# Eight experts ordered by token count, each place with its own matmul width, and weight loads issued ahead of the stores

## The chip, the cores and the metric

One core of a Trainium2 chip runs the whole program. The metric is device time in microseconds (us) of that core; the kernel is timed in several runs, and one more execution is recorded by the hardware profiler. TensorE is called PE here, its weight loads PEld, VectorE DVE, ScalarE ACT, GpSimd POOL, and SyncE, which only issues DMAs, SP.

## What is computed

Three stages follow each other. (1) Retention: for 4 batches, 8 heads, 576 positions and head size 64, decayed scores times `v`; the result is read as N = 2304 tokens of D = 512. (2) A mixture of 8 experts with one expert per token:

```python
e_idx = np.argmax(x @ w_gate, axis=1)
for e in range(E):
    mask = e_idx == e
    h = np.maximum(x[mask] @ w1[e], 0.0)      # 512 -> 1024
    out[mask] = gate_w[mask, None] * eom[mask, e, None] * (h @ w2[e])   # 1024 -> 512
```

(3) A bilinear layer: `((x @ w_a) * (x @ w_b)) @ w_out`, 512 to 1536 to 512.

With the reference's inputs the router's argmax gives the experts 0 to 7 these numbers of tokens: 259, 313, 335, 290, 273, 287, 292, 255 (2304 in all).

## The kernel before

**Precision.** Every f32 product is made of three products of rounded operands: a tile is split in a high part (`w_hi`, `x_hi`, `h_hi`, written by ACT) and the rest (`w_lo`, `x_lo`, `h_lo`, written by DVE), and PE does hi by hi, hi by lo and lo by hi into one PSUM bank.

**Routing (before the experts).** While the retention runs, every token gets a rank within its expert. A table of slots then holds, expert after expert, the token numbers in blocks of R = 112. The experts' columns are worked off in *windows*: a window is up to W = 3 x 112 = 336 tokens of one expert. DVE counts how many windows each expert needs (`count` against `full`, `n_win`, L1354 to L1356), sums them to `starts` (the first window of each expert, L1361 to L1364), and works out for each window its first slot (`win_slots`) and its first output column (`win_cols`, L1377 to L1391). PE, ACT, DVE, POOL and SP read `starts` into registers, and loop over the windows of each expert; a window's number of columns is always 336, whether or not the expert fills it, and what is computed too much is overwritten by the next window's result. With the counts above every expert needs one window, so there are 8; they are numbered from 0.

**The experts.** The loops go over pairs of experts (`pair_of_experts`, L465), since the weights have two buffers, s = 0 and 1. For window b of expert e:

- PE (`body`, L1885): first layer, 8 blocks f of the hidden size, 4 blocks d of D, three products each: 96 matmuls of 336 columns (L1895, L1903 for the first three f, which are interleaved, and L1913 for the other five), then the second layer, 96 more (L1924). Behind blocks 2 to 5 of the second layer it transposes the next window's tokens, three transposes each (`turn_window`, L1869), into `px`. Before transposing block d it waits for `x_lo` of block d - 1. Block f of the first layer uses the bank of block f - 3, and waits for `h_lo` of that block.
- ACT (`body`, L945) and DVE (`body`, L1427) each run one fixed order: five blocks of `h_hi` (L954) / `h_lo` (L1436); then, in turn, one unit of the *next* expert's weights (`w_hi`, L950 / `w_lo`, L1431, 1024 columns) and one of the remaining three blocks, and a fourth unit; then four more units in turn with the next window's `x_hi` (L931) and `x_lo` (L1406). DVE's unit in that part comes behind its `x_lo`, ACT's comes ahead of its `x_hi`. Last come one part of the bilinear weights, which each window prepares on the side (L977, L1414 to L1425), and the copies of the result to `y_out` (L981, L1461), after which `y_kept` lets SP store and PE write `py` again.
- SP (`body`, L651): when window b has begun, it asks for the 8 units of the next expert's weights (512 KB each, L604), waits until the prepared bilinear weights of the last window are stored, and loads the next raw ones (L622); then it stores the window's token numbers (L669), waits for `y_kept` at the window's end, stores `y_out` (L674) and, once DVE has finished them, the prepared bilinear weights (two DMAs of 896 KB, L628).
- POOL gathers the tokens of the window after the next one from DRAM (L802) when the transposes have freed `x_blk`.

The last expert's window (`last_experts`, `last_body`) has a body of its own, in which ACT and DVE prepare the input of the bilinear stage instead of weights. The first expert's weights are loaded and split during the retention (`first_units`, `first_low`, L1284).

**The bilinear stage** is fully written out: 18 steps, products of 384 columns (L1979) and an output part of 512 columns (L2004).

Of the kernel before, what the change touches and what calls it, by code (L numbers as in the profile page):

```python
# [5 lines left out]
def retention_table(heads, seq, chunk, scale):  # L6
# [10 lines left out]
    return np.stack([q, k], 1)[..., order].reshape(chunk, 2, chunks * heads).astype(np.float32)  # L17


def retention_moe_bilinear(nc, q, k, v, w_gate, w_output_gate, w1, w2, w_a, w_b, w_out, out):  # L20
# [5 lines left out]
    i32 = mybir.dt.int32  # L26
    u32 = mybir.dt.uint32
    ALU = mybir.AluOpType
# [18 lines left out]

    R = 112
    WB = 3
    W = WB * R  # L50
    NJ = -(-N // W)
    NW = (N + E * (W - 1)) // W
    NB = WB * NJ
# [35 lines left out]
    CONSTS = 27  # L89
# [8 lines left out]
    gate_dram = nc.dram_tensor("gate_of_token", (N, 1), f32, kind="Internal").ap()  # L98
    powers_dram = nc.inline_tensor(retention_table(H, S, P, DH ** -0.5), name="decay_powers").ap()
# [3 lines left out]
    with ctx:  # L103
# [55 lines left out]
        starts = sb("starts", [1, E + 2], i32)  # L159
        win_cols = sb("win_cols", [1, NW1], i32)  # L160
# [18 lines left out]
        n_win = sb("n_win", [P, E], on=phase)  # L179
# [12 lines left out]
        full = sb("full", [P, NJ], on=phase)  # L192
# [25 lines left out]
        count = sb("count", [P, E, NJ], on=phase)  # L218
        st_f = sb("st_f", [P, E + 1], on=phase)
        st_x = sb("st_x", [P, E + 1, E], on=phase)  # L220
# [98 lines left out]
        powers_in = sem("powers_in")  # L319
        const_in = sem("const_in")  # L320
# [135 lines left out]
        def expert_windows(eng, e, s, b0, body):  # L456

            body(e, s, b0, True)
            b1 = eng.value_load(starts[0:1, bass.ds(e + 1, 1)], min_val=1, max_val=NW - 1 + s)
            with eng.If(b1 > b0 + 1):  # L460
                with eng.Fori(b0 + 1, b1) as b:
                    body(e, s, b, False)
            return b1

        def pair_of_experts(eng, e, body):  # L465

            b = eng.value_load(starts[0:1, bass.ds(e, 1)], min_val=0, max_val=NW - 1)
            for s in range(2):
                b = expert_windows(eng, e + s, s, b, body)

        def experts(eng, body):

            with eng.Fori(0, E // 2) as pair:
                pair_of_experts(eng, pair * 2, body)


        def last_experts(eng, body, last_body):

            b = eng.value_load(starts[0:1, E - 2:E - 1], min_val=0, max_val=NW - 1)
            b = expert_windows(eng, E - 2, 0, b, body)  # L480
# [53 lines left out]
        def _(sp):  # L534
# [116 lines left out]
            def body(e, s, b, first):  # L651

                if first:
# [3 lines left out]
                    for u in range(UE):  # L657
                        load_unit(e + 1, 1 - s, u)
# [1391 lines left out]
```

## Time and profile before

| | |
|---|---|
| median of 3 runs | 791.69 us (790.98 to 793.42) |
| the profiled execution's own time | 791.41 us |
| its span in the trace | 789.6 us |
| PE busy | 776.4 us, 98% of the span |
| PEld / DVE / ACT / POOL busy | 718.6 / 479.3 / 282.0 / 78.8 us |
| experts, first matmul to last | 121.1 us to 368.6 us of the span |

The page gives for each engine its busy time, in 40 slices how busy it was and which clock PE was granted, then the chain of work that ended last, and the costliest groups of instructions. The trace behind it can be asked for single instructions in order of time, for what each waited for, and for sums over a stretch. A PE instruction's listed duration overlaps with the next one's; what counts for the time is the distance from start to start.

### The profile page before, as it was taken

The page shows a single profiled execution, that of the slowest core. Times are in us where ns is not written, and L with a number is a line of the kernel's source. Part 1 is how long each engine was busy: PE and PEld are TensorE (multiplying, and loading weights), DVE is VectorE, ACT ScalarE, POOL GpSimd, SP SyncE. Part 2 cuts the span into 40 slices and gives each one's busy share as a digit, 9 for nine tenths or more (in the row PEclk, how much of TensorE's full clock was granted, in tenths as well). Part 3 has the DMA queues.
Part 4 walks back from the last instruction along what each step waited for, and adds up shares of the span by engine and source line. Part 5 has one row for each costly group of instructions (what it writes and reads, how often), then busy time and mean ns, then how long its engine had stood idle before and what let it go on. Part 6 is the DMA issues. An engine that isn't in the chain of part 4 may idle for free.

```text
span 789.6 us, 15184 instructions
## 1 busy us (share of the span) xinstructions
PE 776.4 (98%) x5483; PEld 718.6 (91%) x5486; DVE 479.3 (61%) x898; ACT 282.0 (36%) x501; POOL 78.8 (10%) x112
## 2 busy tenths in 40 slices
PE   8999999999999999999999999999999999999996
PEld 6888859999999999999899999999999999999994
DVE  5577886655856757656666777654663565444471
ACT  4555644453644544634232233222122222221121
POOL 2000031102102002010002000111100011110002
PEclk9999999999999999999999999999999999999998
DMA  8999738296695695867962458875445556454502
GB/s 180 239 236 244 200 110 262 85 344 216 212 361 176 244 327 176 298 216 260 370 245 81 152 198 345 310 286 202 177 159 210 201 215 238 160 196 149 201 1 80
DMA packets 116594, 169.09 MB, mean 214 GB/s; under 512 B 63965, under 2 KB 83455, under 8 KB 116543
## 3 DMA queue, kind: packets, MB, share of 16 engines
q1 hardware_dynamic: 112223, 157.45, 58.5%
q0 software_dynamic: 4176, 10.92, 4.3%
q8 instruction: 31, 0.51, 0.3%
q14 instruction: 20, 0.16, 0.1%
q10 hardware_dynamic: 144, 0.04, 0.0%
HBM read 131.34 MB, written 37.06 MB: 213 GB/s over the span
## 4 chain that ended last, share of the span: by engine, by line
PE 94%; DMA 2%; POOL 1%; DVE 1%; issue 1%; SPq 0%; ACT 0%; POOLq 0%; DVEq 0%
PE pz L1979 32%; PE po L2004 19%; PE py L1924 15%; PE pu L1913 10%; PE pu L1895 4%; PE pscore L1669 3%; PE pout L1723 2%; PE pu L1903 2%; DMA w_lo<-bilinear_weights 1%; PE pq L1657 1%; PE pq L1683 1%; PE pstate L1711 1%; PE px L1869 1%; PE pk L1657 1%; PE pout L1699 1%; PE pscore L1753 1%
## 5 line engine op out<-in xcount | busy, mean ns | idle before, releaser
L1979 PE MATMUL pz<-x_hi,w_hi 128*128 128x384 f32 x504 | 170.2, 338 | 0.8 <-DMA w_lo<-bilinear_weights 0.8
L1979 PE MATMUL pz<-x_hi,w_lo 128*128 128x384 f32 x504 | 169.6, 337 | 0.0
L1979 PE MATMUL pz<-x_lo,w_hi 128*128 128x384 f32 x504 | 169.2, 336 | 0.0
L1528 DVE TENSOR_TENSOR u<-pz,p 128x384 f32<-128x384 f32 x72 | 40.2, 558 | 115.4 <-PE pz L1979 114.9
L1979 PEld LDWEIGHTS pz<-x_hi,w_hi 128*128 128x128 f32 x504 | 94.5, 187 | 4.3 <-DMA w_lo<-bilinear_weights 1.1
L1979 PEld LDWEIGHTS pz<-x_lo,w_hi 128*128 128x128 f32 x504 | 94.7, 188 | 0.6
L1979 PEld LDWEIGHTS pz<-x_hi,w_lo 128*128 128x128 f32 x504 | 94.6, 188 | 0.0
L1026 ACT COPY p<-pz 128x384 f32<-128x384 f32 x36 | 17.3, 481 | 212.7 <-PE pz L1979 211.0
L1431 DVE TENSOR_TENSOR w_lo<-land,w_hi 128x1024 fp32r<-128x1024 f32 x56 | 68.2, 1217 | 28.9 <-ACT w_hi L950 28.9
L2004 PE MATMUL po<-wo_hi,g_hi 128*128 128x512 f32 x216 | 84.2, 390 | 0.0
L2004 PE MATMUL po<-wo_hi,g_lo 128*128 128x512 f32 x216 | 84.2, 390 | 0.0
L2004 PE MATMUL po<-wo_lo,g_hi 128*128 128x512 f32 x216 | 84.2, 390 | 0.0
L1924 PE MATMUL py<-h_hi,w_hi 128*128 128x336 f32 x256 | 83.7, 327 | 0.0
L1924 PE MATMUL py<-h_hi,w_lo 128*128 128x336 f32 x256 | 81.0, 317 | 0.0
L1924 PE MATMUL py<-h_lo,w_hi 128*128 128x336 f32 x256 | 80.9, 316 | 0.0
L950 ACT CAST w_hi<-land 128x1024 fp32r<-128x1024 f32 x56 | 58.7, 1050 | 26.5 <-DMA land<-in_moe_w_dram 26.5
L1913 PE MATMUL pu<-x_hi,w_hi 128*128 128x336 f32 x160 | 51.5, 322 | 0.0
L1913 PE MATMUL pu<-x_hi,w_lo 128*128 128x336 f32 x160 | 50.7, 317 | 0.0
L1913 PE MATMUL pu<-x_lo,w_hi 128*128 128x336 f32 x160 | 50.6, 316 | 0.0
L1436 DVE SCALAR_TENSOR_TENSOR h_lo<-pu,h_hi 128x336 fp32r<-128x336 f32 x56 | 28.3, 505 | 34.4 <-ACT h_hi L954 33.0
L1041 ACT CAST g_hi<-g 128x384 fp32r<-128x384 f32 x72 | 33.6, 515 | 43.5 <-DVE g L1551 40.2
L1924 PEld LDWEIGHTS py<-h_lo,w_hi 128*128 128x128 f32 x256 | 48.4, 189 | 0.0
(256 smaller groups left out, 1330.7 us busy)
## 6 DMA issues: line engine op xcount, KB each, us to landing
land<-in_moe_w_dram SPq DMA_DIRECT2D x64, 512.0 KB, 8.0
w_hi<-bilinear_weights SPq DMA_DIRECT2D x31, 896.0 KB, 4.6
w_lo<-bilinear_weights SPq DMA_DIRECT2D x31, 896.0 KB, 6.9
bilinear_weights<-w_hi SPq DMA_DIRECT2D x12, 896.0 KB, 6.1
bilinear_weights<-w_lo SPq DMA_DIRECT2D x12, 896.0 KB, 8.2
wo_land<-in_moe_w_out_dram SPq DMA_DIRECT2D x18, 512.0 KB, 3.6
y_columns<-y_out SPq DMA_DIRECT2D x8, 672.0 KB, 5.4
q_in<-in_q_dram SPq DMA_DIRECT2D x32, 128.0 KB, 2.9
```

Of the source, the lines that this page charges most:

```text
L950: nc.scalar.copy(w_hi[1 - s][:, u, :], land[1 - s][:, u, :]).then_inc(hi_done, 1)
L1026: nc.scalar.copy(p1[:], pz[n % 2][:, 0:T]).then_inc(z_kept_act, 1)
L1041: nc.scalar.copy(hi[:, MADE[i], :], g[:, MADE[i], :]).then_inc(g_hi_ready, 1)
L1431: nc.vector.tensor_tensor(w_lo[1 - s][:, u, :], land[1 - s][:, u, :], w_hi[1 - s][:, u, :], ALU.subtract).then_inc(lo_done, 1)
L1436: nc.vector.scalar_tensor_tensor(out=h_lo[:, f, :], in0=pu[f % NPU][:, 0:W], scalar=0.0, in1=h_hi[:, f, :], op0=ALU.max, op1=ALU.subtract) ...
L1528: nc.vector.tensor_tensor(dst, pz[n % 2][:, 0:T], more, ALU.add).then_inc(z_kept_dve, 1)
L1669: last = nc.tensor.matmul(pscore[half][0:r, j, 0:r], kT[d, c, j, 0:r], qT[d, c, j, 0:r], start=True, stop=True)
L1895: last = nc.tensor.matmul(pu[f][:, 0:W], w[s][:, d, at(f)], x_hi[:, d, :], start=(d == 0 and w is w_hi), stop=False)
L1913: last = nc.tensor.matmul(pu[f % NPU][:, 0:W], w, m[:, d, :], start=(d == 0 and n == 0), stop=(d == DC - 1 and n == 2))
L1924: last = nc.tensor.matmul(py[d][:, 0:W], w, m[:, f, :], start=(f == 0 and n == 0), stop=(f == FF - 1 and n == 2))
L1979: ins = nc.tensor.matmul(pz[n % 2][:, 0:T], w, m, start=(k in FRESH and j == 0 and i == 0), stop=(j == DH2 - 1 and i == 2), skip_group_che ...
L2004: ins = nc.tensor.matmul(po[i][:], m[:, c, rows], w_, start=(q == 0 and f == 0 and n == 0), stop=(q == NQ - 1 and f == 1 and n == 2))
```

## The change

Experts are no longer worked off by their number. Each has a *place*: the one whose weights are loaded during the retention, expert 0, comes first, the other seven follow by ascending token count. Each place has a fixed width:

`WIDTH = [320, 272, 288, 296, 300, 304, 320, W]`, with W = 336.

All matmuls of a window, `h_hi`, `h_lo`, `y_out` and the stores of a window have the width of its place instead of 336. The gather, the transposes, and `x_hi` and `x_lo` keep 336. An expert with more tokens than its place's width gets further windows of the same width, each advancing by 224 tokens. DVE works out the places at run time (`key`, `less`, `place_of`, `at_rank`, `by_rank`), with four small tables that ACT's queue loads at the start. The loops over pairs of experts are written out, one body for each place, on all engines.

In SP's order the first 4 units of the next weights now come ahead of the stores of the window before, and the last 4 behind them.

On DVE, one split of a unit (`first_low`) leaves the last batch of the retention (where the fifth row tile's was) and comes behind `starts`; the one behind `starts` and the one behind `gate_t` come behind the `x_lo` of window 0, and PE asks for one unit fewer before its first window.

```diff
+def expert_plan(experts, blocks, widths, step, tokens):
+    order = np.arange(experts)
+    prefer = np.where(order == 0, -8.0 * experts * tokens, order)
+    more = 1 + -(-(tokens - min(widths)) // step)
+    over = np.array([[-1] + [w + step * j for j in range(more - 1)] for w in widths])
...
-    NJ = -(-N // W)
-    NW = (N + E * (W - 1)) // W
-    NB = WB * NJ
+    WIDTH = [320, 272, 288, 296, 300, 304, 320, W]
+    STEP = WB - 1
+    NW = E + -(-(N - min(WIDTH)) // (STEP * R))
+    NB = -(-N // R)
...
             def body(e, s, b, first):
                 if first:
                     sp.wait_ge(began, b + 1)
                     sp.sem_inc(alone_sp, 1)
-                    for u in range(UE):
-                        load_unit(e + 1, 1 - s, u)
-                    sp.wait_ge(stage_stored, e * 32 + 32)
-                    sp.sem_inc(alone_sp, 1)
-                    load_raw((w_a, w_b)[s], e - s, 0, stage_in)
-                    sp.wait_ge(cols_ready, 1)
-                    sp.wait_ge(slots_stored, 32)
+                    expert = sp.value_load(order[0:1, e + 1:e + 2], min_val=0, max_val=E - 1)
+                    for u in range(DC):
+                        load_unit(expert, 1 - s, u)
+                    if e == 0:
+                        sp.wait_ge(cols_ready, 1)
+                        sp.wait_ge(slots_stored, 32)
+                    else:
+                        store_y(e - 1, b - 1)
+                        sp.wait_ge(stage_lo_done, e * 2)
+                        store_w2(e - 1, 0, stage_stored)
+                    for u in range(DC, UE):
+                        load_unit(expert, 1 - s, u)
+                    sp.wait_ge(stage_stored, e * 32 + 32)
+                    load_raw((w_a, w_b)[s], e - s, 0, stage_in)
+                elif e < E - 1:
+                    store_y(e, b - 1)
+                store_ids(e, b)
+                if e == E - 1:
+                    store_y(e, b)
...
-                    unit = None if last and c == TOGETHER else first_units(b, c - 1 if not (last and c > TOGETHER) else c - 2, first, last)
+                    unit = None if last and c >= TOGETHER else first_units(b, c - 1, first, last)
...
-            first_low(UE - 2, UE - 2)
+            first_low(3, 5)
...
-            first_low(UE - 1, UE - 1)
...
             for d in range(DC):
                 turn_window(0, d, py[d])
+            for u in range(UE - 2, UE):
+                first_low(u, u)
...
-            pe.wait_ge(lo_done, UE - 1)
+            pe.wait_ge(lo_done, UE - 2)
             def body(e, s, b):
+                cols_of = slice(0, WIDTH[e])
...
-                            last = nc.tensor.matmul(py[d][:, 0:W], w, m[:, f, :],
+                            last = nc.tensor.matmul(py[d][:, cols_of], w, m[:, f, cols_of],
                                                     start=(f == 0 and n == 0), stop=(f == FF - 1 and n == 2))
```

How the instructions stand on SP, in a window in the middle (`land0` is the buffer of the next expert's weights, `w2_land0`, `w2_hi0` and `w2_lo0` the bilinear weights prepared on the side). Before:

```order
L604 ISA [waits began]
L604 DMA land0<-in_moe_w1_dram 128x1024
...
L604 DMA land0<-in_moe_w2_dram 128x2x512
...
L622 DMA w2_land0<-in_moe2_w_b_dram 128x2x128 [waits stage_stored]
...
L669 DMA token_of_column<-token_of_slot 16x21
L671 ISA [waits y_stored]
L674 DMA y_columns<-y_out 128x4x336 [waits y_kept_act,y_kept_dve]
...
L628 ISA [waits stage_lo_done]
L628 DMA bilinear_weights<-w2_hi0 128x1792
...
L628 DMA bilinear_weights<-w2_lo0 128x1792
```

And now, in window 1:

```order
L703 TENSOR_LOAD order [waits began]
...
L628 DMA land0<-in_moe_w1_dram 128x1024
...
L692 REGISTER_ALU [waits y_kept_act,y_kept_dve]
L692 DMA y_columns<-y_out 128x4x320
L652 DMA bilinear_weights<-w2_hi0 128x1792 [waits stage_lo_done]
L652 DMA bilinear_weights<-w2_lo0 128x1792
...
L628 DMA land0<-in_moe_w2_dram 128x2x512
...
L646 DMA w2_land0<-in_moe2_w_b_dram 128x2x128 [waits stage_stored]
...
L682 DMA token_of_column<-token_of_slot 16x17
```

The stores, which stood ahead of all 8 loads of a window (as the last rows of the window before), now stand between its first 4 and its last 4, and the raw bilinear weights stay last.

On DVE, between the last rank of the retention stage and `starts` (`tokens_of` is in `plog`). Before:

```order
L1354 TENSOR_TENSOR count<-plog,full 128x56
L1356 TENSOR_REDUCE n_win<-count 128x8 [waits dve_step]
L1358 TENSOR_SCALAR slots<-pout 128x3 [waits slots_done,dve_step]
...
L1361 TENSOR_TENSOR st_x<-earlier,n_win 128x72
L1362 TENSOR_REDUCE st_f<-st_x 128x9 [waits dve_step]
L1363 TENSOR_SCALAR starts<-st_f 1x1 [waits dve_step]
L1364 CAST starts<-st_f 1x9
```

And now:

```order
L1404 TENSOR_TENSOR less<-key 1x64 [waits dve_step]
L1407 TENSOR_SCALAR slots<-pout 128x3 [waits slots_done,dve_step]
...
L1410 TENSOR_REDUCE place_of<-less 1x8
L1411 TENSOR_TENSOR at_rank<-win_no,place_of 1x64 [waits dve_step]
L1413 TENSOR_TENSOR by_rank_x<-at_rank,of_expert 1x192 [waits dve_step]
L1415 TENSOR_REDUCE by_rank<-by_rank_x 1x3x8 [waits dve_step]
L1417 TENSOR_TENSOR count<-by_rank,over 1x88 [waits dve_step]
L1418 CAST order<-by_rank 1x8 [waits dve_step]
L1419 TENSOR_REDUCE n_win<-count 1x8
L1420 TENSOR_TENSOR st_x<-earlier,n_win 1x72 [waits dve_step]
...
L1423 CAST starts<-st_f 1x9
```

Ahead of the `slots` three small steps stand where two stood; between the `slots` and `starts` there are seven more steps.

## Rows read from the trace of the kernel before

**Rows 1.** The page: engines, granted clock in 40 slices, chain that ended last.
```profile
PE 776.4 (98%) x5483; PEld 718.6 (91%) x5486; DVE 479.3 (61%) x898; ACT 282.0 (36%) x501; POOL 78.8 (10%) x112
PEclk9999999999999999999999999999999999999998
PE 94%; DMA 2%; POOL 1%; DVE 1%; issue 1%; SPq 0%; ACT 0%; POOLq 0%; DVEq 0%
```

**Rows 2.** Busy time by stage: stretch, its length, busy by engine, PEclk, DMA share, GB/s.
```profile
121.10:368.60 247.50, 247.46 (x1631) 246.00 (x1632) 153.21 (x222) 119.41 (x192) 29.49 (x32) 1.00 0.71 249
```

**Rows 3.** Chain that ended last, window 2: start, us, engine, line, count.
```profile
183.32 3.68 PE pu L1895 x24
187.00 1.84 PE pu L1903 x12
188.84 9.40 PE pu L1913 x60
198.24 5.55 PE py L1924 x36
203.79 0.29 PE px L1869 x3
204.08 1.85 PE py L1924 x12
...
210.52 3.70 PE py L1924 x24
```

**Rows 4.** The same chain in the bilinear stage.
```profile
506.63 8.20 PE po L2004 x36
491.95 14.69 PE pz L1979 x84
```

**Rows 5.** A row of PE's timeline in the retention stage, and its group by form.
```profile
100.02 0.66 PE L1683 MATMUL pq<-ident,xT 128*128 128x128 f32 x4
...
L1683 PE MATMUL pq<-ident,xT 128*128 128x128 f32 x64 | 10.5, 287 | 0.0
```

**Rows 6.** ACT's timeline in window 2 (start, us; idle before and releaser in brackets).
```profile
187.65 0.45 ACT L954 ACTIVATE h_hi<-pu 128x336 fp32r<-128x336 f32 x1 [2.55 <-PE pu L1903]
197.32 1.05 ACT L950 CAST w_hi<-land 128x1024 fp32r<-128x1024 f32 x1 [4.15 <-DMA land<-in_moe_w_dram]
204.12 0.44 ACT L931 CAST x_hi<-px 128x336 fp32r<-128x336 f32 x1 [0.53 <-PE px L1869]
```

**Rows 7.** DVE's timeline, end of window 2 and start of window 3.
```profile
203.06 1.21 DVE L1431 TENSOR_TENSOR w_lo<-land,w_hi 128x1024 fp32r<-128x1024 f32 x1
204.59 0.51 DVE L1406 TENSOR_TENSOR x_lo<-px,x_hi 128x336 fp32r<-128x336 f32 x1 [0.32 <-ACT x_hi L931]
211.46 1.23 DVE L1431 TENSOR_TENSOR w_lo<-land,w_hi 128x1024 fp32r<-128x1024 f32 x1
216.53 0.91 DVE L1461 COPY y_out<-py 128x336 f32<-128x336 f32 x2
219.07 1.12 DVE L1436 SCALAR_TENSOR_TENSOR h_lo<-pu,h_hi 128x336 fp32r<-128x336 f32 x2 [1.63 <-ACT h_hi L954]
```

**Rows 8.** SP's timeline in window 2.
```profile
186.66 0.43 SPq L674 DMA_DIRECT2D y_columns<-y_out  x1
187.99 1.20 SPq L628 DMA_DIRECT2D bilinear_weights<-w_lo  x1
192.74 4.68 SPq L604 DMA_DIRECT2D land<-in_moe_w_dram  x8
```

**Rows 9.** DMA of window 2: total, then stretches as in rows 2.
```profile
DMA packets 3841, 7.94 MB, mean 256 GB/s; under 512 B 320, under 2 KB 1856, under 8 KB 3840
...
188.00:192.00 4.00, 4.00 (x27) 3.87 (x26) 2.03 (x4) 1.46 (x4) 0.00 (x0) 1.00 1.05 401
208.00:214.00 6.00, 6.00 (x43) 5.99 (x42) 4.92 (x9) 2.56 (x4) 1.43 (x3) 1.00 0.00 0
```

**Rows 10.** Timelines of DVE, PE and the chain, end of the routing to the first window.
```profile
105.11 1.21 DVE L1284 TENSOR_TENSOR w_lo<-land,w_hi 128x1024 fp32r<-128x1024 f32 x1
118.27 0.16 DVE L1390 TENSOR_REDUCE early_n<-early 1x1 f32<-1x15 f32 x1
118.46 0.14 DVE L1391 TENSOR_SCALAR first_group<-early_n 1x1 int32<-1x1 f32 x1
119.85 1.23 DVE L1284 TENSOR_TENSOR w_lo<-land,w_hi 128x1024 fp32r<-128x1024 f32 x1
121.04 1.75 DVE L1406 TENSOR_TENSOR x_lo<-py,x_hi 128x336 fp32r<-128x336 f32 x4
...
116.66 3.51 DMA x_blk<-x_tokens,slots
121.14 3.98 PE pu L1895 x24
```

More of the change, by code:

```diff
@@ L17, in retention_table @@
     return np.stack([q, k], 1)[..., order].reshape(chunk, 2, chunks * heads).astype(np.float32)
+def expert_plan(experts, blocks, widths, step, tokens):
+    import numpy as np
+    order = np.arange(experts)
+    prefer = np.where(order == 0, -8.0 * experts * tokens, order)
+    more = 1 + -(-(tokens - min(widths)) // step)
+    over = np.array([[-1] + [w + step * j for j in range(more - 1)] for w in widths])
+    of_expert = np.stack([0 * order, order, blocks * order])
+    by_rank = np.zeros((3, experts + 1))
+    by_rank[2, experts] = blocks * experts
+    return more, [np.asarray(m, dtype=np.float32).reshape(1, -1) for m in (prefer, over, of_expert, by_rank)]
 def retention_moe_bilinear(nc, q, k, v, w_gate, w_output_gate, w1, w2, w_a, w_b, w_out, out):
@@ L1011, in last_body @@
                     act.wait_ge(y_stored, b * 16 + 16)
-                    nc.scalar.copy(y_out[:, d, :], py[d][:, 0:W]).then_inc(y_kept[0], 1)
-            with act.Fori(0, E // 2 - 1) as pair:
-                pair_of_experts(act, pair * 2, body)
-            n_windows = last_experts(act, body, last_body)
+                    nc.scalar.copy(y_out[:, d, 0:w], py[d][:, 0:w]).then_inc(y_kept[0], 1)
+            n_windows = experts(act, body, last_body)
             act.wait_ge(down_done, n_windows * DC)
@@ L1512, in last_body @@
                     dve.wait_ge(y_stored, b * 16 + 16)
-                    nc.vector.tensor_copy(y_out[:, d, :], py[d][:, 0:W]).then_inc(y_kept[1], 1)
-            with dve.Fori(0, E // 2 - 1) as pair:
-                pair_of_experts(dve, pair * 2, body)
-            n_windows = last_experts(dve, body, last_body)
+                    nc.vector.tensor_copy(y_out[:, d, 0:w], py[d][:, 0:w]).then_inc(y_kept[1], 1)
+            n_windows = experts(dve, body, last_body)
             def keep_sum(step, kind, k, dst, more, of):
@@ L1894, in up_first @@
                             for w in (w_hi, w_lo):
-                                last = nc.tensor.matmul(pu[f][:, 0:W], w[s][:, d, at(f)], x_hi[:, d, :],
+                                last = nc.tensor.matmul(pu[f][:, cols_of], w[s][:, d, at(f)], x_hi[:, d, cols_of],
                                                         start=(d == 0 and w is w_hi), stop=False)
```

161 lines of the change are left out of this document (95 added, 66 removed).

## The prediction

> **What bounds the kernel now.** I read the page first [rows 1]: PE is busy for 98% of the span, its granted clock reads 9 tenths or more in every slice but the last (the 2.4 GHz level), and 94% of the chain that ended last is PE. So only work that leaves PE, or a new wait on PE, moves the time. The table by stage [rows 2] gives the experts 247.5 us, 247.46 of them PE busy, over eight windows: 30.9 us each. The chain through one window [rows 3] has nothing but PE: 3.68 + 1.84 + 9.40 + 5.55 + 3 x 1.85 + 3.70 = 29.72 us for 192 matmuls of 336 columns, or 154.8 ns each from start to start, and four groups of transposes of 0.29 us. No other engine holds PE up there: ACT waits 4.15 us for weights in the middle of the window [rows 6] and PE does not notice.
>
> **What a column costs.** The bilinear stage has two more widths on the same chain [rows 4]: 84 matmuls of 384 columns take 14.69 us, 174.9 ns each; 36 of 512 columns take 8.20 us, 227.8 ns each. From 336 to 384 that is 20.1 ns for 48 columns, 0.419 ns each; from 384 to 512, 52.9 for 128, 0.413. One column in one cycle at 2.4 GHz is 0.417, and about 15 ns a matmul are fixed. The three widths lie on one line, so at 336 the columns set the spacing and not the weight load that each matmul has. I extend the line down to 272 columns: 154.8 - 64 x 0.417 = 128.1 ns. The nearest row that says whether loads can follow is four f32 transposes with a 128x128 load each [rows 5]: (0.66 - 0.29) / 3 = 0.123 us apart. A full load every 123 ns has been seen, and 128 is asked.
>
> **The narrower windows.** With the counts of the reference the places hold 259, 255, 273, 287, 290, 292, 313 and 335 tokens, against widths of 320, 272, 288, 296, 300, 304, 320 and 336: each fits, there are still 8 windows. The widths sum to 2436, before 8 x 336 = 2688. That is 252 columns fewer in each of 192 matmuls: 252 x 192 x 0.417 ns = **20.2 us less** (20.0 with 0.413, 20.3 with 0.419). It is all on PE, which is the path. The shortest window falls from 30.9 to 25.8 us.
>
> The Trainium skill speaks against this size: TensorE: Matmul & The Clock Gate, section Back-to-back issue gap, gives a sustained spacing of about 81 ns at 128 columns and 131 ns at 512, 0.13 ns a column. By that the change would be worth 6.3 us. This trace disagrees at 512 columns (227.8 ns), and the sum goes by the trace.
>
> **What now has to fit in a shorter window.** The cover of every transfer and split shrinks by up to 5.1 us. I take window 1 (272 columns), with T its start on PE.
>
> *DVE and ACT, middle.* DVE's splits of a unit (1.23 us) alternate with `x_lo` (0.51), which stay at 336 columns [rows 7]; overlapped starts make that about 1.65 us a round. PE's round there was 1.85 + 0.29 = 2.14 us and becomes 1.83. Tight but covered. In the first layer DVE's round is 1.55 to 1.65 against PE's 1.54; PE asks for these blocks only five blocks later, so I cost it at nothing. Without that cover it would be 0.1 us a block.
>
> *DVE, end.* The bilinear splits and `y_out` follow the last unit. That last unit starts at 211.46 and `y_out` ends at 217.44 [rows 7]; its start is tied to the last transposes, and those come only 60 matmuls ahead of the window's end. With 272 columns 60 matmuls shrink by 1.6 us in all, of which 36 spacings and one round fall ahead of it: the end of `y_out` moves from 3.3 to about 3.9 us behind the next window's start. The first `h_lo` of that window is wanted 4.97 us behind its start now (219.07 against 214.1), about 4.4 with 288 columns. The 1.63 us that DVE waited there shrink to about 0.5, and it still has to read `starts` and branch, which is hidden now. I take 0.1 us for each short window; bounds 0, and 1 us for the three shortest if the branch shows.
>
> *PE's own start.* PE asks for `h_lo` of block 0 after 36 matmuls, and that needs 28 matmuls, ACT (0.45) and DVE (0.51). The 8 matmuls between shrink from 1.24 to 1.02 us while ACT and DVE shrink less (0.45 to 0.41, 0.51 to about 0.43): under 0.1 us a window. With the item above: **+0.5 us** over the stage, bounds 0 and 3.
>
> *The weights.* Before, SP asked for them at T + 9.4 (192.74 against 183.3), behind three stores [rows 8], and the first was used at T + 14 [rows 6]. DMA moves 7.94 MB a window at 401 GB/s when it runs, and stands idle for the last 6 us [rows 9]. If only the width had changed, DVE's fourth split would still end at T + 21 (203.06 + 1.21 [rows 7]) where the next `x_lo` is wanted near T + 17.8, and PE would stand some 2 to 3 us in the narrowest windows. The new order on SP asks for 4 units (2.10 MB) at about T + 1, so the first lands long before ACT wants it (T + 8.4, five blocks in). What is late next is unit 4, behind the stores: what is left of the gather (0.69 MB at most), 2.10, `y_out` 0.66, bilinear stores 1.84 and the unit itself 0.52 make 5.8 MB, 14.5 us at 401 GB/s, so T + 15.5, and T + 13.8 if the gather is over. ACT must have split it (1.05 us) before the `x_hi` behind the first transposes, which come 132 matmuls in: 20.5 us in before (203.79 against 183.32), 17.0 now. So unit 4 is wanted by T + 16.3 in window 1 and between T + 17.2 and 18.9 in windows 2 to 6; units 5 to 7 follow at 1.3 us each where 1.83 us are available. Cost: nothing, with 0.8 us to spare in window 1. The raw bilinear weights wait for the stores (about T + 13.5) and land near T + 21, wanted at T + 25. Each window's work is 7.9 MB or 20 us of DMA, in 25.8 us at the least.
>
> **Routing.** One split of 1.13 us leaves the rank's path [rows 10]; the ranks then wait for PE's logits, so about 0.45 us of it come back, and the gather of window 0 (3.51 us of DMA on the chain) starts that much earlier. DVE gets seven more small steps before `starts`, about 0.2 us each (118.27 to 118.46), +1.4 us, and one more for `hop`; but the split at 119.85 (1.2 us) moves behind `x_lo`. So `x_lo` of window 0 stays at about 121.0, and is first wanted 24 matmuls in; `starts` is wanted by PE at 115.2 and comes at about 115.1, before fillers that the gather outlasts. Sum: **-0.4 us**, bounds -0.8 and +1. The four small loads on ACT's queue at the start come before a table load, and ACT's first real work is at 6.2 us: nothing. Last window and bilinear stage are as before: 0.
>
> **The sum.** 791.41 (the profiled execution) - 20.2 + 0.5 - 0.4 = 771.3. The median is 0.28 above that execution, so 771.6 us. About 0.3% (2.4 us) is what a measurement of this kernel can tell from no change.
>
> **The rivals.**
> 1. *The last four units, or DVE, come too late.* For it: under 1 us to spare in window 1, DVE rounds within 0.2 us of PE's, a stretch of DMA at full rate 20 us long. Against: windows 2 to 6 have 2 to 3 us to spare. If unit 4 lands at T + 17.5 only windows 1 and 2 lose, 1.2 and 0.3 us; at T + 19.5 the six windows lose 11 us. With the DVE bound of 3 us I put this case at 773.5 to 780.
> 2. *The weight load gets a floor below 336 columns.* PEld is listed busy for 246.0 of 247.5 us [rows 2], and no row has such loads at 128 ns behind f32r matmuls; the 123 ns are transposes. A floor of 141 ns, halfway, would cost (12.9 + 6.2 + 2.9 + 1.2) ns x 192 = 4.5 us: 776. A floor at 154.8 would leave nothing: 792. The skill's rule quoted above is of this kind, with a gain of 6.3 us; the line through three widths is against it.
> 3. *Slower: one expert more than fits.* From one token over its place's width an expert runs a second window of that width, 25.8 to 30.9 us, which is more than the 20 gained: 797 to 802. The narrowest margins are 1 token at the last place (where before had the same limit) and 7 to 17 at places 1 to 6; before never counted against these widths, so the trace does not show them. The counts above are exact sums of the reference's choice, and a near tie moves one token or two.
> 4. *The change does not do what it says:* the split order on SP hides nothing because the stores at its middle wait for `y_kept` (T + 3.9). SP is through with its 4 loads at about T + 3.5, so this wait costs 0.4 us of issue while 2 MB are queued: no time of its own.
>
> **How the numbers follow.** The forecast (770.3 to 773.5) gets 0.74, rival 1 0.17, rival 2 0.05 (0.01 of it with no gain), rival 3 0.03, and something faster than 770.3 0.01. Two in ten may stay out; I take 769.7 to 778.0, which holds the forecast, its bounds and most of rival 1. Faster by over 0.3%: 0.96; within: 0.01; slower: 0.03.
>
> **What would show it.** The experts' stretch takes about 227.5 instead of 247.5 us, PE busy all through. On the chain, 60 first-layer matmuls of a 272-column window take 7.8 us (9.40 at 336): a spacing of 128 ns; more means rival 2. ACT's wait for the first unit (4.15 us) is gone, and a wait for `land` may stand at the fifth unit; PE idle at the transposes (`px`) with `x_lo` as the releaser means rival 1. More than 8 x 32 matmuls of each product in the second layer means rival 3. The first window starts near 120.7 us. The forecast is wrong if windows 1 to 4 are longer than 192 x spacing + 1.3 us.

## The result and the profile after

The changed kernel takes 785.65 us (median of 5 runs, 783.74 to 788.01) against 791.69 for the kernel before (790.62 to 793.42), a ratio of 0.9918 (95% interval 0.9891 to 0.9945; intervals stand in brackets from here on). 6 us were gained where 20 were forecast. The profiled execution took 783.74 us; its span is 781.9 us, 7.7 less than before.

The page of the changed kernel: span, engines, granted clock in 40 slices, chain that ended last.

```profile
span 781.9 us, 14929 instructions
PE 760.1 (97%) x5485; PEld 700.4 (90%) x5485; DVE 479.5 (61%) x906; ACT 280.7 (36%) x500; POOL 75.3 (10%) x110
PEclk9999999999999999999999999999999999999999
PE 79%; DMA 10%; SPq 4%; issue 2%; DVE 2%; ACT 1%; POOLq 0%; POOL 0%; DVEq 0%
```

PE's busy time fell by 16.3 us, but PE no longer fills the chain: it was 94% of it [rows 1] and is 79%, and DMA is on it with 10%. The table by stretch has one row for each of windows 0 to 6 (columns as in [rows 2]):

```profile
122.92:152.64 29.72, 29.72 (x204) 29.48 (x205) 20.19 (x30) 14.44 (x24) 4.90 (x7) 1.00 0.57 183
152.64:180.08 27.44, 25.93 (x207) 25.42 (x205) 18.46 (x28) 15.06 (x24) 3.03 (x4) 1.00 0.81 289
180.08:211.03 30.95, 28.68 (x207) 28.28 (x206) 19.45 (x29) 15.00 (x24) 3.34 (x5) 0.94 0.74 254
211.03:239.91 28.88, 27.76 (x206) 27.36 (x205) 19.41 (x29) 15.10 (x24) 3.21 (x4) 1.00 0.77 272
239.91:268.81 28.90, 28.44 (x207) 27.81 (x205) 19.38 (x29) 15.15 (x24) 3.21 (x4) 1.00 0.80 274
268.81:297.97 29.16, 28.25 (x207) 27.85 (x205) 19.42 (x29) 15.17 (x24) 3.22 (x4) 1.00 0.79 271
297.97:329.08 31.11, 29.79 (x206) 29.36 (x205) 19.68 (x30) 15.27 (x24) 3.30 (x5) 1.00 0.73 254
sum 206.16, PE 198.58 PEld 195.55 DVE 135.99 ACT 105.18 POOL 24.22; mean PE 28.37 PEld 27.94 DVE 19.43 ACT 15.03 POOL 3.46
```

Read the length against PE's busy time. In window 0 they are equal. In each of the six others PE stands for 0.5 to 2.3 us, 7.58 in all; before, the same seven windows took 216.65 us, all of them busy. Window 2 also has a granted clock of 0.94 in the mean. The list of PE's waits in these windows has one line (total, times, longest), and it is the sign of rival 1:

```profile
PE px L1934 <- DVE x_lo L1466: 7.5, 6, 2.3
```

What is behind it shows on the chain through window 2 (T = 180.08), and on ACT's timeline:

```profile
186.59 13.56 DMA land<-in_moe_w_dram
...
201.12 0.44 ACT x_hi L975
201.58 0.52 DVE x_lo L1466
202.10 0.04 issue
202.15 0.82 PE px L1934 x3
```

```profile
193.55 1.05 ACT L996 CAST w_hi<-land 128x1024 fp32r<-128x1024 f32 x1
200.16 1.04 ACT L996 CAST w_hi<-land 128x1024 fp32r<-128x1024 f32 x1 [5.57 <-DMA land<-in_moe_w_dram]
201.12 0.43 ACT L975 CAST x_hi<-px 128x336 fp32r<-128x336 f32 x1
```

ACT has split units 0 to 3 by 194.6 and then waits 5.57 us for unit 4, the first behind the stores. The transposes that its next `x_hi` copies were done at 198.3. ACT cannot take them first, because its program has the unit ahead of them; `x_lo` waits for `x_hi`, and PE's second transposes for `x_lo`.

SP's timeline and the DMA by stretch, in the same window:

```profile
181.22 2.48 SPq L628 DMA_DIRECT2D land<-in_moe_w_dram  x4
184.81 0.42 SPq L692 DMA_DIRECT2D y_columns<-y_out  x1
185.28 0.50 SPq L652 DMA_DIRECT2D bilinear_weights<-w_hi  x1
185.84 0.53 SPq L652 DMA_DIRECT2D bilinear_weights<-w_lo  x1
186.59 4.97 SPq L628 DMA_DIRECT2D land<-in_moe_w_dram  x4
```

```profile
180.08:183.10 3.02, 3.02 (x25) 3.02 (x24) 2.82 (x4) 1.62 (x3) 2.07 (x3) 1.00 0.58 119
183.10:186.70 3.60, 3.60 (x28) 3.43 (x27) 2.28 (x6) 1.24 (x3) 0.00 (x0) 1.00 0.95 344
186.70:190.00 3.30, 3.30 (x27) 3.30 (x27) 1.09 (x3) 1.76 (x3) 0.00 (x0) 1.00 1.02 302
190.00:196.00 6.00, 6.00 (x48) 6.00 (x47) 5.83 (x7) 4.05 (x6) 0.00 (x0) 1.00 1.05 400
196.00:200.00 4.00, 3.88 (x30) 3.64 (x29) 0.00 (x0) 0.00 (x0) 0.00 (x0) 1.00 1.02 392
...
202.20:205.50 3.30, 3.30 (x15) 3.30 (x16) 2.66 (x3) 1.74 (x3) 0.00 (x0) 0.50 0.50 135
```

SP asks at T + 1.1 as forecast. The DMA engines are full only from T + 3 (share 0.58 before that, 119 GB/s), and for the next 7 us they move 344 and 302 GB/s although they are full; only then come the 400 of [rows 9]. The last row is the other thing to see: behind the 2.27 us in which PE stood, the granted clock is 0.50, PE's lower level, for 3.3 us.

The rest of the difference lies outside these windows. The first window starts at 122.92 instead of 121.14 [rows 10], and the part from window 7 to the end takes 452.8 us instead of 451.8.

### The profile page after: what moved, and what is told of

It reads as the page before. It is cut to its first block, busy times and chain, and to the rows that moved or that the text cites. A ratio compares the mean times of both kernels' runs of the same rounds, so it can differ in the third digit from the quotient of the medians.

```text
span 781.9 us, 14929 instructions
## 1 busy us (share of the span) xinstructions
PE 760.1 (97%) x5485; PEld 700.4 (90%) x5485; DVE 479.5 (61%) x906; ACT 280.7 (36%) x500; POOL 75.3 (10%) x110
## 4 chain that ended last, share of the span: by engine, by line
PE 79%; DMA 10%; SPq 4%; issue 2%; DVE 2%; ACT 1%; POOLq 0%; POOL 0%; DVEq 0%
PE pz L2047 33%; PE po L2072 19%; DMA land<-in_moe_w_dram 10%; PE py L1992 9%; PE pscore L1734 3%; PE pu L1981 2%; PE pout L1788 2%; SPq L628 2%; PE pq L1748 1%; PE pq L1722 1%; PE pstate L1776 1%; PE px L1934 1%; PE pout L1764 1%; PE pu L1963 1%; PE pk L1722 1%
## 5 line engine op out<-in xcount | busy, mean ns | idle before, releaser
L1992 PE MATMUL py<-h_hi,w_hi 128*128 128x320 f32 (+6 forms) x256 | 80.8, 316 | 0.0
L1992 PE MATMUL py<-h_lo,w_hi 128*128 128x320 f32 (+6 forms) x256 | 77.9, 304 | 0.0
L1992 PE MATMUL py<-h_hi,w_lo 128*128 128x320 f32 (+6 forms) x256 | 77.9, 304 | 0.0
L996 ACT CAST w_hi<-land 128x1024 fp32r<-128x1024 f32 x56 | 58.5, 1046 | 30.1 <-DMA land<-in_moe_w_dram 30.1
L1981 PE MATMUL pu<-x_hi,w_hi 128*128 128x320 f32 (+6 forms) x160 | 49.2, 308 | 0.0
L1992 PEld LDWEIGHTS py<-h_hi,w_hi 128*128 128x128 f32 x256 | 48.8, 191 | 0.0
L1992 PEld LDWEIGHTS py<-h_hi,w_lo 128*128 128x128 f32 x256 | 48.7, 190 | 0.0
L1981 PE MATMUL pu<-x_lo,w_hi 128*128 128x320 f32 (+6 forms) x160 | 48.4, 303 | 0.0
## 6 DMA issues: line engine op xcount, KB each, us to landing
bilinear_weights<-w_lo SPq DMA_DIRECT2D x12, 896.0 KB, 10.7
```

Source lines behind the costliest of these rows:

```text
L996: nc.scalar.copy(w_hi[1 - s][:, u, :], land[1 - s][:, u, :]).then_inc(hi_done, 1)
L1981: last = nc.tensor.matmul(pu[f % NPU][:, cols_of], w, m[:, d, cols_of], start=(d == 0 and n == 0), stop=(d == DC - 1 and n == 2))
L1992: last = nc.tensor.matmul(py[d][:, cols_of], w, m[:, f, cols_of], start=(f == 0 and n == 0), stop=(f == FF - 1 and n == 2))
```

## The experiments

Theory A: unit 4 lands too late for windows this short, and ACT's fixed order hands that on to PE. Rival B: the rounds of DVE or ACT, or the new order itself, are what a short window can't hold. Rival C: the routing and the fillers ahead of the first window (fillers are matmuls on `idle_in` whose results nobody reads; `wait_busy` issues them so that PE does not stand). Rival D: the falls of the clock. A "way" below is the time from the first `slots` on DVE to the first `pu` on PE, 8.38 us before, 9.36 in the changed kernel. The seven windows are windows 0 to 6.

### w336: the old width, all else new

```diff
-    WIDTH = [320, 272, 288, 296, 300, 304, 320, W]
+    WIDTH = [W] * 8
```

> The changed kernel with every place 336 columns wide again, its order of work and its order on SyncE kept. Theory A (the fifth of the eight weight units lands too late for the shortened windows, ScalarE works in a fixed order and holds x_hi back behind it, and PE stands at the transposes): with 30.9 us windows the unit is wanted at T + 20 to 20.5 and lands before, so every window is 30.9 to 31.1 us and PE has no wait there. What is left against the kernel before is the longer routing: first window 0.5 to 2 us later. 791.5 to 793.5 us. Rival B (the new order itself, or the DMA traffic it makes, costs time whatever the width): windows of 31.5 us and more, 795 us and up. Rival C (the start costs nothing by itself): 791 us or less.

794.66 us, ratio 1.0019 [1.0002, 1.0036]. The median lies 1.2 us above the range expected, the windows are as expected. The seven by the table, with no wait of PE in them:

```profile
125.58:342.19 216.61, 216.61 (x1428) 215.31 (x1429) 139.31 (x198) 107.50 (x168) 24.60 (x31) 1.00 0.71 246
```

216.61 us, before 216.65: the new order costs nothing where the window is long. ACT splits unit 4 at T + 18.7 to 20.2 in windows 1 to 6 here too, so the landing is not late because windows are short. It was no earlier in the kernel before, T + 18.9 to 19.9 in the same windows. Its row of window 2 (T = 183.16):

```profile
202.54 1.05 ACT L950 CAST w_hi<-land 128x1024 fp32r<-128x1024 f32 x1 [0.28 <-DMA land<-in_moe_w_dram]
```

Moving units 0 to 3 ahead of the stores brought them forward, but unit 4 has the same stores and the same four units queued ahead of it in either order. 30.9 us had room for that. B falls as far as the order goes. What the kernel pays, about 2 us in the medians (1.5 by the ratio), lies outside the windows: the part from window 7 to the end takes 452.7 us (before 451.8), and the rest is ahead of the first window. In the profiled execution, the slowest of twelve, that window starts at 125.58. PE stood 2.00 us for `starts` ahead of it, and then:

```profile
120.30:123.60 3.30, 3.30 (x11) 1.70 (x10) 2.99 (x16) 0.00 (x0) 0.00 (x0) 0.51 0.29 74
```

The clock falls over the fillers, and the way takes 11.0 us.

### ahead0: all loads behind the stores, as before

```diff
-                    for u in range(DC):
+                    for u in range(0):
                         load_unit(expert, 1 - s, u)
...
-                    for u in range(DC, UE):
+                    for u in range(0, UE):
                         load_unit(expert, 1 - s, u)
```

> The changed kernel with all eight weight loads behind the stores again, as in the kernel before, and the narrow widths kept. Theory A: the units land in the old rhythm, the fourth is split on VectorE near T + 20 to 21, and the next x_lo is wanted at T + 17.8 in the 272-column window; the last four follow about as late as now or a little earlier, since nothing else of the load moves. Windows 1 to 6 are then about as long as now or longer: excess over their columns 8 to 16 us in sum, 783 to 790 us. If the new order on SyncE does all that it is for, this run is over 4 us slower than the changed kernel; if it does nothing, within 2 us of it.

790.96 us, ratio 0.9981 [0.9964, 0.9998], about 5 us over the changed kernel and 1 us above the range expected. The seven windows take 213.15 us, and PE's waits grow:

```profile
PE px L1937 <- DVE x_lo L1469: 11.8, 6, 2.8
```

Now ACT waits 6.02 us for the first unit (window 1, T + 14.4). The change's order on SP, with its loads in two halves, is worth 7 us of windows; without it the narrow columns would have kept 3.5 of the 21.2 us that they save (`early_b` below).

### swap: ScalarE copies x_hi ahead of the unit

```diff
                 for d in range(DC):
-                    high(DC + d)
                     turn_window(b + 1, d, px)
+                    high(DC + d)
```

> The changed kernel with one thing moved on ScalarE: in the rounds of the last four units each x_hi is copied before the unit's rounding, not behind it. Theory A: x_hi no longer waits for the unit of its own round, so a landing up to one round (1.8 us) later is borne; of the 9.6 us by which windows 1 to 6 exceed their columns, about 6 to 8 go, and the longest of PE's waits for x_lo go with them. 776 to 779 us. Rival B (VectorE's rounds of 1.7 us, or PE itself, set the windows): no change, 783 to 786 us. Rival D (a fall of the granted clock to 1.2 GHz makes part of it): 1 to 2 us stay in the window in which it shows.

781.03 us, ratio 0.9851 [0.9827, 0.9876]: 4 to 5 us less from one line. The seven windows take 202.47 us. The expectation of 776 to 779 was missed, since the wait has only moved on by a round:

```profile
PE px L1934 <- DVE x_lo L1466: 5.9, 5, 3.1
```

`x_hi` of the first round is now copied in time, but DVE too has a fixed order, `x_lo` of round 1 behind the `w_lo` of unit 4. And unit 4 was split at T + 20.0 to 20.9, in window 1 at T + 20.9 instead of 18.4. There the first 3 us of DMA moved 117 GB/s and not 196, and the 6 us from T + 6.4 on 353 and not 406. That is 0.56 MB or 1.4 us at 400 GB/s; the rest is not accounted for. `after2` below has T + 19.3 there with the changed kernel itself, so how much of the later landing is due to the moved line is open. Window 6, 320 columns wide, has no wait left.

### early: units 0 to 3 asked for one window earlier

```diff
+            def load_early(e, b):
+                sp.wait_ge(up_done, b * FF)
+                sp.sem_inc(alone_sp, 1)
+                sp.wait_ge(hi_done, e * UE + (UE + DC))
+                sp.sem_inc(alone_sp, 1)
+                expert = sp.value_load(order[0:1, e + 2:e + 3], min_val=0, max_val=E - 1)
+                for u in range(DC):
+                    load_unit(expert, e % 2, u)
...
+                    if e > 0:
+                        sp.wait_ge(hi_done, e * UE + UE)
+                        sp.sem_inc(alone_sp, 1)
+                    for u in range(DC, UE):
+                        load_unit(expert, 1 - s, u)
+                    if e > 0:
                         store_y(e - 1, b - 1)
```

The second hunk stands where the change loads units 0 to 3; `load_early` is called behind each window's body, up to the last but two. So two things move: units 0 to 3 go one window earlier, and units 4 to 7 ahead of the stores; `early_b` moves only the first.

> The changed kernel with the loads of units 0 to 3 asked for in the window before, when its first layer is through and their buffers are free, and units 4 to 7 at the window's start ahead of the stores. Theory A: all eight units land before they are wanted (units 4 to 7 by about T + 11 to 12), the raw bilinear weights last, near T + 21 to 23 where T + 25 is wanted. Excess over the columns 0.5 to 2 us in sum, no ScalarE wait for a landing over 1 us, 774 to 777 us. Rival B (VectorE or PE set the windows): no change, 783 to 786 us. If the raw bilinear weights become late instead, VectorE's waits for them grow and 2 to 5 us of the gain are gone.

774.74 us, ratio 0.9766 [0.9743, 0.9789]. ACT's waits for `land` are gone (30.1 us in the changed kernel, 0.0 here), and so is every wait of PE at the transposes. The seven windows:

```profile
sum 195.96, PE 195.53 PEld 194.18 DVE 135.23 ACT 104.41 POOL 24.74; mean PE 27.93 PEld 27.74 DVE 19.32 ACT 14.92 POOL 3.53
PE pu L1996 <- DVE h_lo L1516: 0.4, 1, 0.4
```

10.2 us came back by moving transfers alone, four of them into the time when DMA stood idle. With the same engines, columns and orders on ACT and DVE, rival B is out. The one wait left is of another kind: the raw bilinear weights land last, DVE ends late, and `h_lo` of window 3 is late by 0.4 us.

### after2: the changed kernel once more

> The changed kernel itself once more, beside the others of this call. 784 to 787 us. Windows 1 to 6 should again exceed their columns by 9 to 11 us in sum, since this follows from the order of the transfers; what should differ from one execution to the next is where the granted clock falls to half for 3.4 us, 0 to 1.5 us each.

786.45 us (782.81 to 792.02), ratio 0.9929 [0.9906, 0.9952]. The seven windows take 206.06 us with 7.7 us of PE's waits: their sum repeats to 0.1 us, though single windows differ by up to 2.3 us.

### ahead8: all eight units ahead of the stores

```diff
-                    for u in range(DC):
+                    if 8 > DC and e > 0:
+                        sp.wait_ge(hi_done, e * UE + UE)
+                        sp.sem_inc(alone_sp, 1)
+                    for u in range(8):
                         load_unit(expert, 1 - s, u)
...
-                    for u in range(DC, UE):
+                    for u in range(8, UE):
                         load_unit(expert, 1 - s, u)
```

> The changed kernel with all eight weight units asked for at the window's start, ahead of y_out and of the bilinear stores. Theory A (what delays unit 4 are the 2.5 MB of stores queued ahead of it): ScalarE's wait for unit 4 goes, unit 4 is there by T + 13, no PE wait for x_lo. The raw bilinear weights, which wait for the stores, move from T + 20 to T + 25 and later, so the last splits and y_out of a window end later and hold up the first h_lo of the next: 2 to 6 us in sum. 778 to 784 us. Rival E (unit 4 is late because transfers run slower than 0.4 MB a us, whatever their order): it still lands behind T + 16, and the time stays at 783 us or more.

779.69 us, ratio 0.9836 [0.9811, 0.9862]. As theory A says, unit 4 is split at T + 13.8 in window 1 and no transposes are waited for. Rival E of the expectation, a late unit 4 in whatever order, is out, though its premise, under 0.4 MB a us, holds for the first 10 us of window 2 in the changed kernel. The price is on the other side. Window 6, and PE's waits:

```profile
293.19:326.86 33.67, 31.23 (x206) 30.94 (x205) 20.56 (x32) 15.72 (x25) 3.21 (x5) 0.95 0.71 242
PE pu L1984 <- DVE h_lo L1504: 4.6, 3, 2.4
```

The raw weights, queued behind the stores, were asked for at 289.75 in window 5 and landed at 294.80, 1.6 us behind the start of window 6. DVE began their splits 1.04 us later, waiting for nothing that the profile shows, and made `h_lo` only after their splits. Behind that idle stretch the clock fell again (0.95 in the mean).

### early_b: units 0 to 3 early, units 4 to 7 behind the stores

```diff
                     if e > 0:
+                        store_y(e - 1, b - 1)
+                        sp.wait_ge(stage_lo_done, e * 2)
+                        store_w2(e - 1, 0, stage_stored)
                         sp.wait_ge(hi_done, e * UE + UE)
                         sp.sem_inc(alone_sp, 1)
                     for u in range(DC, UE):
                         load_unit(expert, 1 - s, u)
-                    if e > 0:
-                        store_y(e - 1, b - 1)
-                        sp.wait_ge(stage_lo_done, e * 2)
-                        store_w2(e - 1, 0, stage_stored)
```

(against the kernel of `early`)

> As the run with units 0 to 3 asked for one window earlier, but units 4 to 7 behind the stores again. In that run windows 3 and 7 began their second layer 0.5 and 0.9 us late, because the raw bilinear weights landed late. Theory A: stores through by T + 9, units 4 to 7 by T + 14 to 16, raw weights right behind the stores' end and no longer late; excess over the columns still none. 773 to 775 us. If units 4 to 7 are late again in the 272-column window, it gets longer than 25.8 us by what they miss.

773.10 us, ratio 0.9761 [0.9737, 0.9785]. All windows are without a wait:

```profile
126.43:321.90 195.47, 195.47 (x1428) 194.22 (x1429) 136.37 (x198) 104.95 (x168) 24.42 (x31) 1.00 0.80 270
```

That is 21.18 us less than before, with PE busy in all of it. The profiled execution was the slowest of six (776.46): its clock fell over the fillers, and its way took 11.0 us.

### early_f6: fewer fillers

```diff
-            wait_busy(12)
+            wait_busy(6)
```

(against `early`)

> As the run with units 0 to 3 asked for one window earlier, with 6 instead of 12 matmuls of filling on TensorE ahead of the first window. In both profiles of the narrow kernel without a fall of the clock there, the way from the slots to the first first-layer matmul takes 9.4 us against 8.4 before. If the fillers are what lengthens it (theory C), about 1 us goes: 773 to 774.5 us. If the gather of the first window ends last anyway, nothing changes: 774 to 775.5 us. If fewer fillers let the clock fall ahead of the window, 775.5 us and more.

776.00 us, ratio 0.9792 [0.9767, 0.9817]. The way shrank as expected, to 8.73 us, but the time did not. Window 6 took 33.52 us instead of 29.60. Its chain, and the table by stretch around PE's idle time:

```profile
288.12 1.58 DMA w_land<-in_moe_w_b_dram
289.70 1.74 issue
291.44 0.43 DVE w_land L1491
...
296.15 0.49 DVE h_lo L1516
```

```profile
293.97:296.60 2.63, 0.15 (x2) 0.00 (x0) 2.51 (x6) 1.85 (x6) 0.00 (x0) 0.91 0.81 271
296.70:299.50 2.80, 2.80 (x10) 2.80 (x11) 0.72 (x2) 0.00 (x0) 0.00 (x0) 0.50 0.95 348
```

The raw weights are late (289.70, T + 1.0 of the next window), and DVE begins their splits only 1.74 us later, in which it waits for nothing that the profile shows ("issue"). The splits and `y_out` stand ahead of `h_lo`, PE idles 2.6 us and then runs at the lower clock. In `early` the same splits began at T + 0.1, right behind the landing, and in the seven windows PE waited for `h_lo` only once, 0.4 us. So the chain has no slack there, and 0.9 us of landing and 1.7 us on DVE decide. Why DVE began late, here and in `ahead8`, is open. In `early_b`, which asks for the raw weights 12.7 us into window 1 and not 18.5, DVE never waits for them. None of the three cases of the expectation foresaw this.

### fill and best: fillers ahead of the read of starts

```diff
-            wait_busy(5)
+            wait_busy(13)
             pe.wait_ge(starts_ready, 1)
...
-            wait_busy(12)
+            wait_busy(4)
```

(`fill` against the changed kernel, `best` against `early_b`)

> The changed kernel with the same 17 filling matmuls ahead of the first window, but 13 of them (was 5) before TensorE reads starts and 4 (was 12) behind. TensorE stood 2.0 us before that read; in three of nine profiles so far the clock fell to half for 3.41 us right behind that idle stretch and the way from the slots to the first window took 11.0 instead of 9.4 us. Theory C (the later starts cost time only through fillers that follow it): the way takes 8.4 to 8.8 us and has no fall of the clock on it; the median falls by 1 to 2 us from that of the changed kernel, 784 to 785.5 us. If the gather ends last, it stays at 9.4.

> Units 0 to 3 asked for one window earlier, units 4 to 7 behind the stores, and the fillers moved as in the run beside. Windows as in that kernel (195.5 us for the first seven, against 206.1 in the changed kernel), the way from the slots to the first window 8.4 to 8.8 us. 772 to 773 us. If the fall of the clock has nothing to do with the idle stretch at starts, it is as before: 773 us and up to 776 in single executions.

`fill`: 784.26 us, ratio 0.9893 [0.9859, 0.9926]. `best`: 773.48 us (770.88 to 777.50; 772 to 773 were expected), ratio 0.9750 [0.9720, 0.9781]. PE's timeline ahead of the first window, in the changed kernel and in `best`:

```profile
117.82 2.75 PE L1842 MATMUL pscore<-idle_in 128*128 128x512 bf16 x12 [1.99 <-issue]
```

```profile
116.55 1.02 PE L1856 MATMUL pscore<-idle_in 128*128 128x512 bf16 x4 [0.27 <-issue]
...
119.87 0.60 PE L1955 MATMUL py<-ident,x_blk 112*128 112x112 f32 x4 [0.66 <-DMA x_blk<-x_tokens,slots]
```

In the changed kernel no transpose waits for the gather: PE stood 1.99 us for `starts`, and 12 fillers of 0.22 us came on top. With most fillers ahead of the read the wait is 0.27 us, the last transposes wait for the gather again, and the way is 8.63 and 8.52 us. So theory C's 0.8 us is in the profiles. In the medians it does not stand out: the intervals of `fill` and `after2` overlap, as do those of `best` and `early_b`.

## Why the prediction was wrong

In the terms of the sum, profiled execution against profiled execution: 771.3 forecast, less 1.5 (the columns, and the short waits at a window's start, came better), plus 10.7 (the weights and what their lateness brings), 2.2 (ahead of the first window), 1.0 (bilinear stage), is 783.7.

**Columns: right, and a little small.** `early_b` and `best` show the windows without anything in the way: 21.2 us less where 20.2 less 0.5 were forecast. The chain of `best` in the 272-column window:

```profile
150.69 3.02 PE pu L1977 x24
...
155.21 7.80 PE pu L1995 x60
163.01 4.54 PE py L2006 x36
```

7.80 us for 60, as forecast, and 4.54 / 36 = 126 ns for those of the second layer, against 154 before [rows 3]: 28 ns for 64 columns, 0.44 each. Rival 2, the floor of the weight load, fell. By the rule of the Trainium skill (TensorE: Matmul & The Clock Gate, section Back-to-back issue gap) the columns were worth 6.3 us, an estimate from its two figures. The measured gain of the change is near that figure, and yet the rule is not what made it so: the spacing fell by three times as much as the rule gives, and the rest was lost elsewhere. A total that fits is no evidence for a cause.

**Waits at the window's start, +0.5: nothing.** PE is busy in all of the 195.47 us of `early_b`.

**The weights: this step failed.** "Cost: nothing, with 0.8 us to spare in window 1" rested on unit 4 landing at T + 15.5. It was split at T + 18.4 in window 1 and T + 19.0 to 21.1 in windows 2 to 6, where T + 16.3 to 18.9 was wanted. In window 2 it came at T + 20.1. The first stretch accounts for 1 us: the 3.02 us hold 0.36 MB, where 401 GB/s from T + 1.1 on would have moved 0.77. The rates of 344 and 302 GB/s in the next 7 us account for 1.3 us against 401 ((3.6 x 57 + 3.3 x 99) / 401). The table to T + 19.9 holds 6.6 MB where the step counted 5.8; this is 1.9 us. The difference must be for the most part units 5 to 7, asked for right behind unit 4. The three make 4.2 of the 4.6 us. The 401 GB/s were the best four microseconds of the trace before, used as if they held from the first one. The same rows could have said so: `y_out`, the stores and the first unit (0.66 + 1.84 + 0.52 MB) were asked for from 186.66 on, and ACT had the unit at 197.32 [rows 6, 8], 3.0 MB in 10.7 us. At that rate 5.8 MB put unit 4 at T + 21.5. The trace before also had the date itself: its unit 4, with the same transfers ahead of it, was split at T + 18.9 to 19.9 (`w336` above), though SP's first request stood at T + 3.5 there, not at T + 1.1.

Second, the step treated lateness as local. It costs PE time only since ACT and DVE take units and blocks in a fixed order (`swap`), and PE's idle time then brings a stretch at the lower clock. Of the 10.7 us PE stood 7.6; of the 3.1 in which it counts as busy 1.7 are the half clock in window 2. The other 1.4 are for the most part listed durations that run on into a wait: in window 1 the last matmul before the wait starts at 171.18 and the next one at 172.97, 1.79 us later where 0.13 is usual, and only 1.51 are listed as idle. Rival 1 was this mechanism, with its price ("at T + 19.5 the six windows lose 11 us"), but it got 0.17, and the range stopped at 778.

**Routing, -0.4: +1.8.** The removed split gave back 0.52 us, near the 0.45 forecast (`slots` at 112.24 in `ahead0`, 112.76 before; ACT's copy `x_tok` of the fifth row tile stands at 105.38 and 105.37 in the two). But the seven steps of DVE took 1.9 us together, 0.07 to 0.38 us each, not 1.4, and `starts` came at 116.7, not 115.1. "Before fillers that the gather outlasts" was the wrong sentence: the fillers start only behind the wait, so its 2 us were not hidden in them, and the gather was outlasted. That is +1.0. The other 1.3 us arose at the very start, where the changed kernel ran a stretch at the lower clock (the table by stretch of the changed kernel, then of the kernel before):

```profile
7.60:11.00 3.40, 3.33 (x22) 3.14 (x23) 1.87 (x3) 0.17 (x1) 0.00 (x0) 0.50 1.33 221
```

```profile
7.60:11.00 3.40, 3.12 (x50) 2.86 (x52) 2.33 (x5) 1.47 (x4) 0.00 (x0) 1.00 1.05 237
```

22 matmuls against 50 in the same 3.4 us. The first copy `x_tok` on ACT comes at 16.22 us, before at 14.90, and the copies stay 1.3 us late up to 106.70. Of the ten profiles of the experiments only `w336` has this stretch at the start, `after2` and `early_b` run 19 and 20 matmuls in it at the full clock, the other seven 49 to 56. The first `slots` stand between 112.24 and 115.53 us in the eleven profiles of the changed kernel and its variants, 112.76 in the one of before. So this part scatters by 3 us from one execution to the next. The change issues four small loads earlier there; whether they play a part was not tried.

**The bilinear stage, 0: +1.0.** All kernels made from the changed one take 452.6 to 452.9 us from window 7 to the end (`early` 453.6, with DVE late once), before 451.8. The chain shows where most of it sits: the groups of 84 take 14.7 us as in [rows 4], but three take 15.0 (from 506.12, 598.22 and 689.99; before, one took 14.9). In each a weight load of PE waits 0.34 us for DVE's `a_sb`, a sum that reads the bank which the next product writes. In the first of them DVE stands 0.37 us ahead of it, waiting for nothing that the profile shows; before, `a_sb` follows at once there:

```profile
519.24 0.56 DVE L1593 TENSOR_TENSOR a_sb<-pz,u 128x384 f32<-128x384 f32 x1 [0.37 <-issue]
519.85 0.19 PEld L2047 LDWEIGHTS pz<-x_hi,w_hi 128*128 128x128 f32 x1 [0.34 <-DVE a_sb L1593]
```

```profile
527.72 0.56 DVE L1528 TENSOR_TENSOR a_sb<-pz,u 128x384 f32<-128x384 f32 x1
```

The page lists 42 and 29 packets of instructions on the two queues that carry them, before 31 and 20, so the longer program may be the cause; it was not tested.

**The other rivals.** The extra window did not come: the trace has 256 matmuls of each product in the second layer. That the split order does nothing is refuted by `ahead0`. The forecast's own test, "PE idle at the transposes (`px`) with `x_lo` as the releaser means rival 1", named what happened.

Where that leaves the change: as made it gives 6 us, and with units 0 to 3 one window earlier and the fillers moved it gives about 20, at 773.48 us, 0.9750 [0.9720, 0.9781] of the kernel before. The profiled execution of that version took 770.88 us.

## What to carry to other kernels

When a stretch bound by one engine gets shorter, everything in it that keeps its length (transfers, splits) must be dated from the trace, from the request to the landing with all that is queued between, and not by bytes over the best rate seen; [rows 6, 8] had such a date, 3.0 MB in 10.7 us. A new order in a queue brings forward only the transfers that get fewer bytes ahead of them; unit 4 did not get fewer. Ask for a transfer when its buffer comes free, which can be a window before it is needed, and look which transfer becomes the last one then. An engine with a fixed order hands one late input on to all that stands behind it, so look for operands that are ready while their engine waits for something else.

## What the runs showed of the hardware that was not expected

Behind stretches in which TensorE stood, its granted clock was 0.50 for about 3.4 us in several profiles: 2.27 us at the transposes (the changed kernel), 2.00 us at `starts` (`w336`), 2.6 us at `h_lo` (`early_f6`). Each costs up to 1.7 us on top of the wait. It does not follow every such wait: of the nine profiles with 2.0 to 2.1 us idle at `starts`, `w336`, `swap` and `early_b` show it, the changed kernel, `after2`, `early`, `ahead0`, `ahead8` and `early_f6` do not. Nor does the length of the wait decide: in window 2 of `ahead8` it followed 1.8 us, and in window 1 of `swap` PE stood 3.08 us and the clock stayed at 1.00. In `early_f6` it fell 0.5 us before PE restarted, in `w336` 1.3 us after. Together with the scatter at the start this moves the profiled executions of one kernel by microseconds; whether it explains the whole scatter of the medians, and why `best` and `early_b` could not be told apart, was not tested.

The rate of the DMA engines was not one number: full by their share in all of these stretches, they moved 344 and 302 GB/s in window 2 while the gather's queue took 15% and 24% of their time beside the first loads, and 392 to 407 once it was through (windows 1 and 2). In `swap` it was 353 GB/s with 12% for the gather. That the gather is the cause was not tested.
